# Two fused MLPs behind a causal convolution: the residue is written over the denominator, |h| gets a third buffer, and five pieces of work stand elsewhere in the engines' orders

## The reference, cut to what matters

```python
# x (2, 4096, 192), weight (8, 7)
w   = softmax(weight, axis=-1)                     # 8 heads, 7 taps
x   = causal_conv(x, w).reshape(8192, 192)         # each head's 24 channels by its own 7 taps
# first MLP
h   = x @ w_in1                                    # (8192, 2048)
x   = max(0.01 * h, h) @ w_out1                    # (8192, 192)
# second MLP
h   = x @ w_in2
P   = a0 + a1*h + a2*h^2 + a3*h^3
Q   = 1 + |b0| * |h| + |b1| * h^2
out = (P / (Q + 1e-6)) @ w_out2                    # (8192, 192), float32
```

## Time and profile before

| | |
|---|---|
| median of 3 runs | 1379.4 us (1378.86 to 1379.6) |
| the profiled execution | 1378.26 us, its span 1376.5 us |
| TensorE busy (PE) | 1276.2 us, 93% of the span |
| VectorE (DVE) | 1086.2 us, 79% |
| ScalarE (ACT) | 1025.9 us, 75% |
| GpSimd (POOL) | 642.4 us, 47% |
| mean granted TensorE clock | 0.983 |

### The profile page before, as it was taken

The page is one execution under the profiler, slowest core; times in us unless marked ns, Lnnn a source line. Parts: engine busy times, 40 slices in busy tenths (PEclk is TensorE's granted clock), DMA queues, the critical chain, the costliest instruction groups (busy, mean ns, idle before and its releaser), DMA issues.

```text
span 1376.5 us, 14572 instructions
## 1 busy us (share of the span) xinstructions
PE 1276.2 (93%) x5724; PEld 1026.1 (75%) x5724; DVE 1086.2 (79%) x945; ACT 1025.9 (75%) x1027; POOL 642.4 (47%) x265
## 2 busy tenths in 40 slices
PE   7989999999999999999999999999999999999674
PEld 6768777787877878787787877778787777878453
DVE  3568879788787887878888787878878797787775
ACT  4677777887777787777787777788777778777564
POOL 0034544545445454454445454454545445454554
PEclk8999999999999999999999999999999999999887
DMA  5300000000000000000000000000000000000000
GB/s 172 91 1 13 0 25 1 12 13 1 25 1 24 1 12 13 1 24 0 24 1 1 24 0 24 1 12 13 1 24 1 25 1 12 1 1 12 0 12 12
DMA packets 25091, 21.73 MB, mean 16 GB/s; under 512 B 2909, under 2 KB 23997, under 8 KB 25023
## 3 DMA queue, kind: packets, MB, share of 16 engines
q1 hardware_dynamic: 25023, 20.80, 5.1%
HBM read 14.49 MB, written 6.30 MB: 15 GB/s over the span
## 4 chain that ended last, share of the span: by engine, by line
POOL 45%; issue 43%; PE 4%; ACT 4%; DVE 3%; DMA 1%; POOLq 0%; SPq 0%; DVEq 0%; ACTq 0%
POOL den L309 23%; POOL lo L315 23%; PE h L614 2%; ACT rec L347 1%; DVE pol L504 1%; ACT rec L350 1%; PE acc L579 0%; PE acc L633 0%; DMA band<-tap_rows 0%; PE acc L634 0%; DMA tap_rows<-out_cm 0%; DVE lo L518 0%; PE acc L624 0%; DMA coef_b<-in_moe_b 0%; PE acc L626 0%
## 5 line engine op out<-in xcount | busy, mean ns | idle before, releaser
L614 PE MATMUL h<-xs,wa 128*128 128x512 f32 x2520 | 616.3, 395 | 38.4 <-DVE pol L512 25.8
L309 POOL TENSOR_TENSOR den<-den,rec 128x1024 f32<-128x1024 f32 x128 | 322.2, 2517 | 669.1 <-ACT den L385 669.1
L614 PEld LDWEIGHTS h<-xs,wa 128*128 128x128 f32 x2520 | 470.3, 189 | 165.7 <-DVE pol L512 38.5
L315 POOL TENSOR_TENSOR lo<-pol,rec 128x1024 fp32r<-128x1024 f32 x128 | 322.6, 2521 | 55.3 <-DVE pol L504 55.3
L492 DVE SCALAR_TENSOR_TENSOR hi<-pol,coef_a,rec 128x1024 fp32r<-128x1024 f32 x128 | 164.3, 1284 | 137.5 <-ACT rec L350 89.2
L518 DVE TENSOR_TENSOR lo<-h,hi 128x1024 fp32r<-128x1024 f32 x128 | 156.2, 1221 | 102.1 <-ACT hi L394 102.1
L633 PE MATMUL acc<-lo,wb 128*128 128x512 f32 x512 | 203.6, 398 | 33.5 <-POOL lo L315 33.5
L624 PE MATMUL acc<-hi,wb 128*128 128x512 f32 x512 | 206.1, 403 | 16.9 <-issue 15.8
L368 ACT ACTIVATE rec<-h 128x1024 f32<-128x1024 f32 x124 | 127.3, 1027 | 124.1 <-POOL lo L315 71.3
L347 ACT ACTIVATE rec<-den,one 128x1024 f32<-128x1024 f32 x128 | 147.4, 1152 | 80.9 <-POOL den L309 80.9
L498 DVE SCALAR_TENSOR_TENSOR den<-den,hi 128x1024 f32<-128x1024 f32 x128 | 199.6, 1559 | 3.9
(11 more groups left out here) (85 smaller groups left out, 937.4 us busy)
## 6 DMA issues: line engine op xcount, KB each, us to landing
out<-out_tok SPq DMA_DIRECT2D x16, 384.0 KB, 2.6
x_tok<-in_x SPq DMA_DIRECT2D x64, 82.5 KB
pol<-in_moe_w_out SPq DMA_DIRECT2D x4, 384.0 KB, 4.2
x_tok<-in_x SPq DMA_DIRECT2D x16, 78.0 KB
den<-in_moe_w_out SPq DMA_DIRECT2D x3, 384.0 KB, 4.0
den<-in_moe_w_in SPq DMA_DIRECT2D x2, 512.0 KB, 5.2
rec<-in_moe_w_in SPq DMA_DIRECT2D x4, 256.0 KB, 5.5
pol<-in_moe_w_in SPq DMA_DIRECT2D x1, 512.0 KB, 6.0
```

What stands on the lines that cost most here:

```text
L309: nc.gpsimd.tensor_tensor(den[k][:, :], den[k][:, :], rec[k][:, :], ALU.mult).then_inc(s_den, 1)
L315: nc.gpsimd.tensor_tensor(lo2[k][:, :], pol[k][:, :], rec[k][:, :], ALU.mult).then_inc(s_lo2, 1)
L614: last = T.matmul(dst[:, half, :], lhs, xs[m][:, part, :], start=(j == 0), stop=(j == 4))
```

## The change

The residue is written over `den` instead of `pol`, so that POOL reads `den` and `rec` for the lo part. |h| and the reciprocal use three buffers (`RECS`) in turn instead of two. Accordingly |h| waits only for the lo part of pair n - 3, the slope waits for that of pair n - 2 (it overwrites the residue), and the numerator's first step waits for the residue of pair n - 2 (which reads `pol`).

In ACT's order the slope now stands behind |h| (behind `split_xt` in phase 6 and the `out_tok` copies in phase 3) and ahead of `copy_conv` and the numerator's first step. The `out_tok` copies stand ahead of that step too.

In DVE's order `out_moves` comes first in its step; `split_x2` comes between `quotient_hi` and `product`, so that in phase 7 the product is ahead of the polynomial and the residue is directly behind it, ahead of `leaky_lo`; `out_sums` and `copy_conv` come ahead of the residue.

`conv_sb` and `out_tok` become views of one tile, `edge`, and the convolution's copies wait for the store of the block three before. The staging tiles become seven.

```diff
-STAGES = 6
+STAGES = 7
+RECS = 3
-        rec = [sb(f"rec{k}", [P, 2 * COLS]) for k in range(2)]
+        rec = [sb(f"rec{k}", [P, 2 * COLS]) for k in range(RECS)]
-        conv_sb = sb("conv_sb", [CT, CTILES, D])
+        edge = sb("edge", [P, CTILES * D])
+        conv_sb = edge[0:CT, :].rearrange("p (t d) -> p t d", t=CTILES)
-        out_tok = sb("out_tok", [P, SUB, D])
+        out_tok = edge[:, 0:SUB * D].rearrange("p (t d) -> p t d", t=SUB)
...
 # POOL
-                    nc.gpsimd.tensor_tensor(lo2[k][:, :], pol[k][:, :], rec[k][:, :], ALU.mult).then_inc(s_lo2, 1)
+                    nc.gpsimd.tensor_tensor(lo2[k][:, :], den[k][:, :], rec[(n - 1) % RECS][:, :], ALU.mult).then_inc(s_lo2, 1)
...
 # ACT
             def copy_conv(c):
                 act.wait_ge(s_conv, c + 1)
+                wait(act, s_stored, 16 * (c - 2))
...
                     act.wait_ge(s_h2, n + 1)
-                    wait(act, s_lo2, n - 1)
-                    nc.scalar.activation(rec[k][:, :], hidden_2_all(n), ACT.Abs).then_inc(s_abs, 1)
+                    wait(act, s_lo2, n + 1 - RECS)
+                    nc.scalar.activation(rec[n % RECS][:, :], hidden_2_all(n), ACT.Abs).then_inc(s_abs, 1)
                 if phase == XT_AT and n > -LEAD and runs(m0 // STEPS, BLOCKS):
                     split_xt(m0 // STEPS)
-                if runs(n, PAIRS):
-                    nc.scalar.activation(pol[k][:, :], hidden_2_all(n), ACT.Identity, scale=coef_a[:, 3:4],
-                                         bias=coef_a[:, 2:3]).then_inc(s_lin, 1)
                 if phase == OUT_AT and runs(o0, BLOCKS):
...
+                if runs(n, PAIRS):
+                    act.wait_ge(s_abs, n + 1)
+                    wait(act, s_lo2, n - 1)
+                    nc.scalar.activation(den[k][:, :], rec[n % RECS][:, :], ACT.Identity, scale=coef_b[:, 1:2],
+                                         bias=coef_b[:, 0:1]).then_inc(s_slope, 1)
                 if phase == CONV_AT and runs(conv_block(n), BLOCKS):
                     copy_conv(conv_block(n))
                 if runs(n, PAIRS):
-                    k = n % 2
-                    act.wait_ge(s_abs, n + 1)
-                    nc.scalar.activation(den[k][:, :], rec[k][:, :], ACT.Identity, scale=coef_b[:, 1:2],
-                                         bias=coef_b[:, 0:1]).then_inc(s_slope, 1)
+                    wait(act, s_res, n - 1)
+                    nc.scalar.activation(pol[k][:, :], hidden_2_all(n), ACT.Identity, scale=coef_a[:, 3:4],
+                                         bias=coef_a[:, 2:3]).then_inc(s_lin, 1)
...
 # DVE
             def copy_conv(c):
                 dve.wait_ge(s_conv, c + 1)
+                wait(dve, s_stored, 16 * (c - 2))
...
-                V.scalar_tensor_tensor(pol[k][:, :], pol[k][:, :], coef_a[:, 0:1], den[k][:, :],
+                V.scalar_tensor_tensor(den[k][:, :], pol[k][:, :], coef_a[:, 0:1], den[k][:, :],
                                        ALU.add, ALU.subtract).then_inc(s_res, 1)
...
+                if phase == FOLD_AT and runs(o0, BLOCKS):
+                    out_moves(o0)
                 if runs(n - 1, PAIRS):
                     quotient_hi(n - 1)
-                    if not x2:
-                        product(n - 1)
                 if x2:
                     split_x2((n + 1) // STEPS)
-                if phase == FOLD_AT and runs(o0, BLOCKS):
-                    out_moves(o0)
+                if runs(n - 1, PAIRS):
+                    product(n - 1)
                 if phase == XT_AT and n > -LEAD and runs(m0 // STEPS, BLOCKS):
                     split_xt(m0 // STEPS)
-                if runs(n - 1, PAIRS) and not x2:
-                    residue(n - 1)
                 if phase == OUT_AT and runs(o0, BLOCKS):
                     out_sums(o0)
                 if phase == CONV_AT and runs(conv_block(n), BLOCKS):
                     copy_conv(conv_block(n))
+                if runs(n - 1, PAIRS) and not x2:
+                    residue(n - 1)
                 if runs(n, PAIRS):
                     polynomial(n)
                 if runs(n - 1, PAIRS) and x2:
-                    product(n - 1)
+                    residue(n - 1)
                 if runs(m0, PAIRS):
                     leaky_lo(m0)
                     for j in range(*split_with(m0)):
                         split_lo(j)
-                if runs(n - 1, PAIRS) and x2:
-                    residue(n - 1)
```

More of the change, by code:

```diff
@@ L102, in conv_mlp_mlp @@
         one = sb("one", [P, 1])
-        conv_row = conv_sb[:, :, :].rearrange("p a c -> p (a c)")
+        conv_row = edge
         out_row = out_cm[:, :, :].rearrange("p a c -> p (a c)")
@@ L308, in step @@
                     pool.wait_ge(s_slope, n + 1)
-                    nc.gpsimd.tensor_tensor(den[k][:, :], den[k][:, :], rec[k][:, :], ALU.mult).then_inc(s_den, 1)
+                    nc.gpsimd.tensor_tensor(den[k][:, :], den[k][:, :], rec[n % RECS][:, :], ALU.mult).then_inc(s_den, 1)
                 if runs(n - 1, PAIRS):
@@ L346, in step @@
                     act.wait_ge(s_den, n)
-                    nc.scalar.activation(rec[k][:, :], den[k][:, :], ACT.Abs_reciprocal_sqrt,
+                    r = rec[(n - 1) % RECS][:, :]
+                    nc.scalar.activation(r, den[k][:, :], ACT.Abs_reciprocal_sqrt,
                                          bias=one[:, 0:1]).then_inc(s_rsq, 1)
                     act.wait_ge(s_rsq, n)
-                    nc.scalar.activation(rec[k][:, :], rec[k][:, :], ACT.Square).then_inc(s_rec, 1)
+                    nc.scalar.activation(r, r, ACT.Square).then_inc(s_rec, 1)
                 if phase == SPLIT_AT and runs((n + 1) // STEPS, BLOCKS):
@@ L491, in quotient_hi @@
                 wait(dve, s_acc2, n - 1)
-                V.scalar_tensor_tensor(hi2[k][:, :], pol[k][:, :], coef_a[:, 0:1], rec[k][:, :],
+                V.scalar_tensor_tensor(hi2[k][:, :], pol[k][:, :], coef_a[:, 0:1], rec[n % RECS][:, :],
                                        ALU.add, ALU.mult).then_inc(s_hi2, 1)
```

## The result

| | before | after |
|---|---|---|
| median of 4 runs | 1379.13 us (1378.04 to 1379.6) | 1367.51 us (1366.67 to 1368.0) |
| ratio | | 0.9916, 95% interval 0.9899 to 0.9933 |
| profiled execution, its span | 1378.26, 1376.5 us | 1367.87, 1366.0 us |
| PE, DVE, ACT, POOL busy | 1276, 1086, 1026, 642 us | 1273, 1133, 1034, 675 us |
| mean granted TensorE clock | 0.983 | 0.970 |

The kernel became faster by 11.6 us, where 27 were forecast. The time lies above the forecast and its own range (1345 to 1362), and inside the wide one (1344 to 1386). The last line of the table is the one to look at first: the clock, which the prediction had left out of the sum.

A forecast was written before the change was run, and what follows sets the result against it. PE was taken to bound the kernel, with stalls made by DVE's and POOL's order of work. Block gains 0.55 + 0.97 + 0.45 + 0.44 - 0.35, less 0.13, give 1.93; times 14, 27.0: 1352 us, range 1345 to 1362 (wide 1344 to 1386).

The forecast's parts named there:

- the working of x2: Phases 7 and 0: product ahead of polynomial delays phase 0's start, phase 0's stall stays; 0.35 us a block lost.
- phase 4: Convolution copy ahead of residue removes TensorE's 0.75 us wait, 0.2 goes to a new conflict with POOL; gain 0.55.
- phase 2: out_moves ahead of quotient_hi empties the accumulator before TensorE wants it; gain 0.97 us a block.
- phase 3: Earlier out_tok copies and sums end before TensorE needs them; gain 0.45 us a block.
- phase 1: It begins with the backlog gone and costs 9.2 us instead of 9.64; gain 0.44 a block.
- 14 blocks run so: The steady part was read as 14 like blocks of 81.47 us, and the gain per block multiplied by 14.
- The three |h| buffers: On ACT, they move the wait for lo from \|h\| to the slope; priced at 0, bounds 0 and 0.4 a block.
- Moving the linear step back costs nothing in a plain step: ACT's later linear step still lets polynomial end at 8.5, TensorE wanting it at 9.07; 0.55 us of slack.
- The tail: End of the run: small losses in plain and x2 steps, out_moves and out_sums gains; taken as 0, between -3 and +3.
- A: Phase 7: POOL gets in before the product, whose margin is 0.07 us; 2.33 more a block, 1385 us; chance 0.26.
- B: Phase 5: residue loses to POOL there too; the step takes 10.83 instead of 9.2, 1375 us; chance 0.10.
- C: Phase 0: residue isn't held by POOL; 2.3 us less a block, 1320 us; chance 0.04.

The follow-up runs named there:

- e1: Changed kernel with ten extra matmuls by a zero tile in phase 1, ahead of TensorE's wait for the polynomial; 1351.91 us.
- e6: Changed kernel with DVE's order of phase 7 undone (polynomial, product, leaky_lo, residue); 1353.21 us.
- e10: Kernel before, with only DVE's new order of phase 7 (x2 splits, product, polynomial, residue); 1342.93 us, ratio 0.9735.
- e9: Changed kernel with the slope back behind the copies on ACT and \|h\| waiting again for lo of pair n - 2; 1321.78 us.
- e8: Kernel before, with only out_moves put first in DVE's order; 1366.15 us, ratio 0.9907.
- e5: Changed kernel with two tiny unused DVE memsets between the x2 splits and the product in phase 7; 1386.61 us, ratio 1.0059.
- e7: Changed kernel with DVE's residue behind the polynomial in phases 0 to 4; 1333.88 us.
- e2: Changed kernel with DVE's residue behind the polynomial in phase 0 only; 1361.15 us.
- e4: Changed kernel with ACT's linear step directly behind \|h\| again and the slope behind the copies; 1368.1 us.
- e11: Kernel before, with only DVE's copy of the convolution put ahead of residue; 1371.07 us, ratio 0.9933.
- e3: Changed kernel with DVE's residue behind the polynomial in phases 0 to 3; 1329.49 us, ratio 0.9634.

## Why the prediction was wrong

**The step that failed** is in the working of x2, "So the stall of phase 0 stays, and this stretch loses 0.35", and in the sum that took it over at 0.35 us. The wait at the start of phase 1 did stay, with the expected length (2.38 us idle, "about 2.5"). It was priced only by what it had cost before. But before, the idle time of that stretch was in pieces: TensorE waited for lo in phase 0 (0.70 us in the longest piece) and then 1.38 at the start of phase 1. The change removed the first, so the idle time of phase 0 came in one piece. Behind that piece the clock fell in ten of 14 blocks, 1.6 us each. The sum had nothing for this, a loss of 16 us; e1 fills the wait and comes out at 1351.9, where 1352 was forecast. The earlier trace rows show clock 1.00, and the prediction carried that over to a kernel whose idle time lay differently. That 1352 is met so closely is in part luck: without the falls the 14 blocks give 25.2 us and not 27.0, and the start and the tail, taken as 0, add 1.5.

**Point by point.** The gains: phase 4 0.54 (forecast 0.55), phase 2 0.97 (0.97), phase 3 0.44 (0.45), phase 1 0.45 (0.44).

Phases 7 and 0 lost 0.52 (0.35): `polynomial` was later by 0.1 and its restart cost 0.1 of TensorE. The prediction put this loss down to x2's order. e6, without that order, has blocks of the same length (79.4 to 79.7) and takes 9.56 in phase 7, so the linear step's later place is enough for most of it; and alone, in the kernel before, x2's order gains 2.6 a block (e10).

"14 blocks run so" is one too many: the windows of the earlier trace rows span 13 blocks, and the 14th has no convolution to gain from.

The three |h| buffers: the prediction gave 0, as the wait moved to the slope. No run tests this with the slope early; but with the slope late, |h|'s own wait for lo is worth 46 us (e9), since it keeps POOL's den multiply behind residue. "Moving the linear step back costs nothing in a plain step" fits the trace, where phase 2 takes 9.07; phase 7, which isn't plain, pays for it (e6). The early slope costs 0.2 a block in phases 4 and 5, as counted, but the prediction didn't ask what phase 0 would be with a late one and a wait on |h|.

The tail, behind the last x2 copy: 3.2 us less, at the edge of the "between -3 and +3" that was taken as 0; in e8, which changes `out_moves` alone, 2.95. The prediction also counted DVE's copies among the operations that POOL doesn't touch. Their own times bear that out (0.65), but in e1 POOL's recorded lead of 0.40 did not always count when such a copy was running.

**The rivals.** A did not happen, and e5 shows it 0.1 us away. Its 2.3 us in phase 7 were right. Its total, 1385, is near e5's 1386.6 by luck: e5 lies 19.1 us above the changed kernel, where A adds 32.6 to the forecast, since the fall of the clock shifts the race of phase 0. B occurred in no steady block of the changed kernel, but in phase 5 of three blocks of e5 and one of e7 (10.83 to 10.84, where B had 10.83), and its like in phase 6 of one block of e1 and e7. C, residue not held in phase 0, was priced at 1320; e9 brought it about and took 1321.8.

The rule of the Trainium skill (SBUF — State Buffer, "Who interferes with whom"), that the operation issued first keeps the shared port for its whole instruction, agrees with the pairs shown here, in that one runs at 1.2 to 1.3 or 2.4 us and the other is stretched beyond its end. Which one was issued first can't always be told from the recorded starts. By the Trainium skill (Perfetto Trace Analysis, "GPSIMD Engine Instruction") POOL's recorded start lies behind its taking up. The traces agree at small distances: a DVE operation recorded 0.06 ahead of POOL got in (1037.34), one 0.03 ahead did not (1012.79). The prediction's distance of 0.07 was thus closer still. The blocks of e1 in which residue gets in 0.40 behind POOL's recorded start (753.32) are not explained by it.

**What stays open.** Why the clock fell behind some waits and not behind others of the same length: 1.3 to 1.6 us never brought it down in the steady part (before, e5, e6, e7), 1.87 did in the odd blocks of e1 and e7, 2.0 in six of 14 blocks (e2), 2.4 in ten of 14 (the changed kernel), 2.5 in 11 of 14 (e4), 2.8 in 11 of 14 (e5). So the share rises with the length up to 2.5 us, and no run here shows what decides in the single block. Nor why DVE's quotient comes 0.44 late in phase 6 of the eleventh block: it does so at that one step in the changed kernel and in all its variants but e5, and nowhere in the kernel before and its variants (e8, e10, e11), and the two races lost in phase 6 are at that step. Nor what decides phase 4 in e1.

## What to carry to other kernels

When an edit leaves TensorE with one long wait in place of two short ones, read the granted clock of that stretch before the sum is believed: filling the wait with ten null matmuls was worth 15.6 us, and a shorter wait is better still. Where two engines exclude each other, work out who comes up first in every step with extra work; making one of them wait longer can be the gain (46 us for one wait, e9, the clock's part included), and an order with a margin of 0.05 us is not one to leave a kernel in. Run the parts of a bundle by themselves: here the x2 order alone gave 36 us and the whole change, which contained it, 12.

## What the runs showed of the hardware

A DVE operation held by POOL ends 1.08 to 1.09 us after POOL's end in every case of all 14 traces, as if only its start were put off; its recorded time contains the waiting (2.5 to 3.5 instead of 1.22 to 1.28). Where the two recorded starts lie within 0.3 us, DVE lost whenever it was recorded less than 0.05 us ahead, and got in at 0.05 or more; the exception lies outside that range, at 0.40 behind POOL, with a DVE copy just before (e1, e2, e3, e5, e6; none in the changed kernel). The clock's fall acts on the other engines as well: in e5, h2 came 1.1 us later and thereby turned a race between DVE and POOL.
